# Attention, soft mixture of experts and a gated layer on one core: w_in by column blocks, its product inside the layer

## The chip, the cores and the metric

One core of one Trainium2 chip runs the whole program. The metric is the device time of one execution in microseconds (us), the median of several runs. TensorE (PE), VectorE (DVE), ScalarE (ACT), GpSimd (POOL) and SyncE (SP, which only issues transfers here) work side by side and meet at semaphores.

## The reference

Three parts follow one another; the change touches the second's end and the third.

1. Attention over 2 x 8 heads of 768 rows and 64 columns, with a mask from hash bits. Its result, laid out as x (1536 x 512), feeds the next.
2. A soft mixture of 8 experts with 4 slots each, 32 slots in all: `logits = x @ phi`, weights d (softmax over rows) and c (softmax over slots), `slot_input = d.T @ x`, per expert `relu(slot_input[e] @ w1[e]) @ w2[e]` (512 to 1024 to 512), and `x = c @ slot_out`.
3. A gated layer: `h = x @ w_in` (512 to 2048), `g = h * sigmoid(1.702 h)`, `out = g @ w_out` (2048 to 512).

Everything is fp32. Since x has rank 32 after part 2, the kernel never forms it: with slot_out (32 x 512) it makes `G = slot_out @ w_in` (32 x 2048) once, and then h as c times G.

## The kernel before

The attention and the routing run to about 299 us of the profile and are not touched. From there:

**Experts (L777 to L808, to about 340 us).** TensorE makes for each expert an up product (L786), two transposes (L796) and a down product (L805), up two experts ahead. All three use plain fp32, and the up and down products have stationary operands of 32 columns, so that four of them lie side by side in the array, each writing 32 of the 128 partitions of PSUM. ScalarE takes the hidden rows out (L960), VectorE rectifies them into hid_t (L1154). After the down products of experts 3, 4 and 5 (TURNS) a turn of c is put in: four transposes (L816) turn c, repeated four times over the partitions, into a bank; ScalarE rounds it into c_t (L970), and VectorE replaces the lower 64 partitions by the bank less its rounded value (L1166). So c_t holds rounded values in its first two quarters of 32 partitions and remainders in the last two.

**Rounded operands.** The products of the output layer take operands in a rounded form of fp32 (F32R), which TensorE takes in one pass. A value is split into a rounded part and a remainder, and sums of products of parts stand in for the exact product. g_stack (128 x 2048) holds G's rounded part in quarters 0 and 2 and its remainder in 1 and 3, against c_t's order, so one product over 128 partitions gives all four combinations.

**G (L834 to L849).** acc, the sum of the down products in four quarters, goes through ScalarE (L972), is summed over the quarters and turned by four small products with stack_i (L834) and copied by VectorE into out_t (L1168: 128 x 4 x 32). Then 16 products in plain fp32 (four chunks of w_in's rows, four blocks of 512 columns) make G, the block j in quarter j of bank 5:

```
            for c in in_order:
...
                for j in range(NQ):
                    last = nc.tensor.matmul(ps[j * QUAD:(j + 1) * QUAD, 5, :], out_t[:, c, :],
                                            win_sb(c)[:, j * BANK:(j + 1) * BANK], start=(c == in_order[0]),
                                            stop=(c == in_order[-1]))
```

VectorE rounds it (L1172) and makes the remainder (L1174). place_g (L412) copies a block's rounded part into two quarters of g_stack (ScalarE) and its remainder into the other two (VectorE), 32 partitions each; block 0 before the layer starts, blocks 1 to 3 in the layer's first three steps.

**The output layer (L852 to L887).** 48 steps s: three groups g of 512 rows, 16 blocks fi of 128 columns of h. up(s) (L859) is one product of g_stack and c_t into bank fi % 4, issued three steps ahead. ScalarE makes the sigmoid (L989), VectorE the gate (L1205), its rounding (L1193) and remainder (L1195). Then 12 products (L878, L879, L880; three for each tile tt of 128 rows) add into banks 4 to 7. In the first 16 steps ScalarE also rounds a block of w_out (round_w, L979) and VectorE makes its remainder (split_w, L1181), one step ahead.

**Transfers.** SP issues all of them, in the written order, on one queue. The weights of the experts go through 11 slots of 2 MB; fills 11 to 19 take slots in the order REUSE and wait until the slot's reader is done (hid_ready or down_done). w_in comes in chunks of 128 rows: the fourth early as win_last (1 MB), the first two as fill 16 (2 MB), the third as fill 17 (1 MB); w_out as fills 18 and 19 (2 MB each). The program's instructions stand in the order that is written out for each engine.

The functions that the diff touches, with the profile's line numbers:

Of the kernel before, what the change touches and what calls it, by code (L numbers as in the profile page):

```python
# [36 lines left out]
def kernel_program(nc, q, k, v, proj, phi, w1, w2, w_in, w_out, out):  # L37
# [28 lines left out]
    with ExitStack() as ctx:  # L66
# [74 lines left out]
        win_last = arena[:, W_AT:W_AT + FF]  # L141
# [18 lines left out]
        at[0] = X_AT + 2 * HR + HD  # L160
        g_part = part(2 * FF // NQ).bitcast(F32R).rearrange("p (y n) -> p y n", y=2)
# [22 lines left out]
        g_high = rounded("g_high", ring_at + 4 * SLOT * 4, [P, DEEP, BANK])  # L184
        g_low = rounded("g_low", ring_at + 4 * SLOT * 4 + 4 * DEEP * BANK, [P, DEEP, BANK])
# [43 lines left out]
        win_last_got = sem("win_last_got")  # L229
# [31 lines left out]
        g_steps = sem("g_steps")  # L261
        g_placed = [sem(f"g_placed{y}") for y in range(2)]
# [81 lines left out]
        def win_sb(c):  # L344
            if c == CH - 1:
                return win_last
            return slot[slot_of(WIN0 + c // 2)].rearrange("p (c n) -> p c n", n=FF)[:, c % 2, :]

        def wout_sb(fi):
            return slot[slot_of(WOUT0 + fi // 8)].rearrange("p (f n) -> p f n", n=HD)[:, fi % 8, :]  # L350
# [39 lines left out]
        def fill(eng, n):  # L390
            s = slot_of(n)
            if n < WIN0:
                e, second = divmod(n, 2)
                eng.dma_start(w2_sb(e) if second else w1_sb(e), w2_d[e] if second else w1_d[e])\
                    .then_inc(w_got[s], DMA)
            elif n < WOUT0:
                c = 2 * (n - WIN0)
                chunks = range(c, min(c + 2, CH - 1))
                eng.dma_start(slot[s].rearrange("p (c n) -> p c n", n=FF)[:, 0:len(chunks), :],
                              win_d[:, c:c + len(chunks), :])\  # L400
                    .then_inc(w_got[s], DMA)
            else:
                f = 8 * (n - WOUT0)
                eng.dma_start(slot[s].rearrange("p (f n) -> p f n", n=HD), wout_d[:, f:f + 8, :])\
                    .then_inc(w_got[s], DMA)

        TURNS = (3, 4, 5)

        def place_g(copy, y, j):

            for x in (y, y + 2):
                last = copy(g_stack[x * QUAD:(x + 1) * QUAD, j * BANK:(j + 1) * BANK],  # L412
                            g_part[j * QUAD:(j + 1) * QUAD, y, :])
            return last
# [823 lines left out]
```

## Time and profile before

| | us |
|---|---|
| median of 3 runs | 498.57 |
| lowest, highest | 497.43, 498.71 |
| profiled execution, its own time | 502.64 |
| span of that execution in the profile | 500.8 |

The profiled execution is one run of its own. The span counts from the first to the last instruction recorded; the execution's own time is 1.8 us longer. TensorE's mean granted clock over the span is 0.978 of full.

### The profile page before, as it was taken

The page shows a single profiled execution, that of the slowest core. Times are in us where ns is not written, and L with a number is a line of the kernel's source. Part 1 is how long each engine was busy: PE and PEld are TensorE (multiplying, and loading weights), DVE is VectorE, ACT ScalarE, POOL GpSimd, SP SyncE. Part 2 cuts the span into 40 slices and gives each one's busy share as a digit, 9 for nine tenths or more (in the row PEclk, how much of TensorE's full clock was granted, in tenths as well). Part 3 has the DMA queues.
Part 4 walks back from the last instruction along what each step waited for, and adds up shares of the span by engine and source line. Part 5 has one row for each costly group of instructions (what it writes and reads, how often), then busy time and mean ns, then how long its engine had stood idle before and what let it go on. Part 6 is the DMA issues. An engine that isn't in the chain of part 4 may idle for free.

```text
span 500.8 us, 8465 instructions
## 1 busy us (share of the span) xinstructions
PE 463.7 (93%) x2817; PEld 328.3 (66%) x2817; DVE 292.5 (58%) x582; ACT 229.8 (46%) x476; POOL 108.3 (22%) x194
## 2 busy tenths in 40 slices
PE   3899999999999999999999979967799999999997
PEld 2776666766766667666676634322588888888885
DVE  4477567756666566756665241012998576648661
ACT  1476666666676666666675321101743132112210
POOL 4233245423552255324522000000000000000000
PEclk9999999999999999999999979988799999999999
DMA  6746668666975668656455759999000020002002
GB/s 151 180 127 176 152 172 241 180 177 143 221 216 162 153 192 228 176 162 158 125 190 164 275 198 362 399 409 374 5 0 2 0 85 0 2 11 75 0 0 85
DMA packets 55832, 76.76 MB, mean 153 GB/s; under 512 B 29312, under 2 KB 33280, under 8 KB 55296
## 3 DMA queue, kind: packets, MB, share of 16 engines
q1 hardware_dynamic: 55808, 76.44, 51.0%
q8 instruction: 15, 0.25, 0.2%
q14 instruction: 9, 0.07, 0.0%
HBM read 51.45 MB, written 3.15 MB: 109 GB/s over the span
## 4 chain that ended last, share of the span: by engine, by line
PE 84%; DVE 7%; DMA 6%; ACT 1%; issue 1%; SPq 1%; DVEq 0%; ACTq 0%
PE ps L632 16%; PE ps L656 14%; PE ps L641 11%; PE ps L878 9%; PE ps L879 9%; PE ps L880 9%; DMA ring_lo<-in_moe_w 4%; DVE max_raw L1013 3%; PE ps L618 2%; PE ps L859 2%; PE ps L610 2%; PE ps L786 2%; DVE arena L1007 2%; PE ps L805 1%; PE ps L718 1%
## 5 line engine op out<-in xcount | busy, mean ns | idle before, releaser
L1013 DVE TENSOR_REDUCE max_raw<-ps 128x1 f32<-128x768 f32 x96 | 91.9, 958 | 74.2 <-PE ps L632 71.4
L900 ACT ACTIVATE arena<-ps,neg_max 128x768 f32<-128x768 f32 x96 | 86.6, 902 | 24.6 <-DVE neg_max L1016 24.1
L632 PE MATMUL ps<-stack_b,stack_a 96*128 96x384 f32 (+1 forms) x384 | 95.3, 372 | 1.7 <-ACT arena L900 1.0
L894 ACT COPY arena<-ps 128x384 f32<-128x384 f32 x144 | 64.3, 480 | 68.8 <-PE ps L641 68.8
L632 PEld LDWEIGHTS ps<-stack_b,stack_a 96*128 96x128 f32 (+1 forms) x384 | 65.1, 196 | 39.3 <-issue 36.6
L641 PE MATMUL ps<-ident,arena 128*128 128x128 f32 x576 | 80.5, 276 | 1.0 <-DVE arena L1007 0.6
L878 PE MATMUL ps<-w_high,g_high 128*128 128x512 f32 x192 | 75.8, 395 | 2.9 <-DVE g_low L1195 2.9
L879 PE MATMUL ps<-w_low,g_high 128*128 128x512 f32 x192 | 75.7, 394 | 0.0
L880 PE MATMUL ps<-w_high,g_low 128*128 128x512 f32 x192 | 75.6, 394 | 0.0
L641 PEld LDWEIGHTS ps<-ident,arena 128*128 128x128 f32 x576 | 69.8, 142 | 5.5 <-DVE arena L1007 1.1
L656 PE MATMUL ps<-arena 128*64 128x384 f32 x384 | 72.1, 498 | 0.0
L989 ACT ACTIVATE arena<-ps 128x512 f32<-128x512 f32 x48 | 28.3, 599 | 81.4 <-PE ps L859 81.4
L555 POOL TENSOR_TENSOR high<-arena,ones 128x768 fp32r<-128x768 f32 x15 | 22.0, 1468 | 134.1 <-DVE arena L1025 131.6
L1205 DVE TENSOR_TENSOR arena<-ps,arena 128x512 f32<-128x512 f32 x48 | 33.0, 688 | 21.8 <-ACT arena L989 21.8
L878 PEld LDWEIGHTS ps<-w_high,g_high 128*128 128x128 f32 x192 | 36.6, 191 | 11.0 <-issue 3.3
L880 PEld LDWEIGHTS ps<-w_high,g_low 128*128 128x128 f32 x192 | 36.6, 191 | 7.7
L879 PEld LDWEIGHTS ps<-w_low,g_high 128*128 128x128 f32 x192 | 36.6, 191 | 7.6
L656 PEld LDWEIGHTS ps<-arena 128*64 128x64 f32 x384 | 23.4, 136 | 25.6 <-issue 25.6
L1195 DVE TENSOR_TENSOR g_low<-arena,g_high 128x512 fp32r<-128x512 f32 x48 | 33.2, 693 | 1.7
L610 PE MATMUL ps<-ident,arena 128*128 128x128 f32 x96 | 18.1, 307 | 12.8 <-DMA arena<-in_k 5.0
L558 POOL TENSOR_TENSOR low<-arena,high 128x768 fp32r<-128x768 f32 x15 | 27.3, 1820 | 1.7 <-DMA stack_a<-low 0.5
L1007 DVE COPY arena<-ps 128x384 f32<-128x384 f32 x48 | 26.7, 556 | 0.8 <-PE ps L641 0.4
(119 smaller groups left out, 420.3 us busy)
## 6 DMA issues: line engine op xcount, KB each, us to landing
ring_lo<-in_moe_w SPq DMA_DIRECT2D x12, 1024.0 KB, 5.6
arena<-in_moe_w SPq DMA_DIRECT2D x5, 2048.0 KB, 8.6
ring_lo<-in_moe_w SPq DMA_DIRECT2D x4, 2048.0 KB, 15.8
stack_a<-high SPq DMA_DIRECT2D x32, 192.0 KB, 3.6
stack_b<-high SPq DMA_DIRECT2D x32, 192.0 KB, 3.9
arena<-in_q SPq DMA_DIRECT2D x16, 192.0 KB, 3.6
arena<-in_k SPq DMA_DIRECT2D x16, 192.0 KB, 4.5
arena<-in_v SPq DMA_DIRECT2D x16, 192.0 KB, 2.4
```

The source lines that it names most:

```text
L632: last = nc.tensor.matmul(s_ps[p % 2][:, c, :], a[r][0:used, rows], b[r][0:used, cols], start=(a is stack_a1), stop=(a is stack_a2))
L641: last = nc.tensor.transpose(ring[b][:, j * P:(j + 1) * P], probs[:, p % 2, kt * P:(kt + 1) * P], ident[:, :])
L656: last = nc.tensor.matmul(o_ps[x * D:(x + 1) * D, :], nat_v[:, r, kt, :], probs_t[:, kt, turned(r, x * HALF)[0], :], start=(kt == 0), stop ...
L878: nc.tensor.matmul(ps[:, 4 + tt, :], g_high[:, s % DEEP, rows], w_h, start=(fi == 0), stop=False)
L879: nc.tensor.matmul(ps[:, 4 + tt, :], g_high[:, s % DEEP, rows], w_l, start=False, stop=False)
L880: last = nc.tensor.matmul(ps[:, 4 + tt, :], g_low[:, s % DEEP, rows], w_h, start=False, stop=(fi == FC - 1))
L894: nc.scalar.copy(probs_t[:, b * HALF:(b + 1) * HALF, g, j * P:(j + 1) * P], ring[b].rearrange("p (a s) -> p a s", a=HALF)).then_inc(t_take ...
L900: nc.scalar.activation(probs[:, p % 2, :].rearrange("p (c s) -> p c s", c=2), s_ps[p % 2], ACT.Exp, bias=neg_max[:, r, p:p + 1], scale=SCA ...
L1007: nc.vector.tensor_copy(probs_t[:, HALF:TILES, g, j * P:(j + 1) * P], ring[1].rearrange("p (a s) -> p a s", a=HALF)).then_inc(t_taken[1], 1)
L1013: nc.vector.tensor_reduce(max_raw[:, r, p:p + 1], s_ps[p % 2], axis=AX.XY, op=ALU.max)\
L1195: nc.vector.tensor_tensor(g_low[:, s % DEEP, :], gated[:, s % 2, :], g_high[:, s % DEEP, :], ALU.subtract)\
L1205: nc.vector.tensor_tensor(gated[:, s % 2, :], ps[:, fi % 4, :], sig[:, s % 4, :], ALU.mult)\
```

## The change

w_in is read in four blocks of 512 columns with all its 512 rows (win_first is block 0), each 1 MB, and w_out in four loads of 1 MB, issued in turn behind the last expert's weights. G is made per block: g_parts(j) makes four products, one per chunk of 128 rows, chunk c into quarter c of bank 3, each a sum of its own; ScalarE copies the bank (take_g); g_sum(j) multiplies it with spread, a 128 x 128 matrix of 16 identities of 32 x 32, which adds the four quarters and puts the sum into all four; ScalarE rounds that into g_stack (round_g), and VectorE overwrites the lower 64 partitions with the remainder (low_g). So g_stack now holds rounded values in quarters 0 and 1 and remainders in 2 and 3, and c_t is made to match: rounded in 0 and 2, remainders in 1 and 3, by two subtractions of 32 partitions. Blocks 1 to 3 are made in the layer's first steps: g_parts(j) at the end of step 4(j - 1), g_sum(j) in the middle of the next. h uses three banks instead of four, and up is issued two steps ahead, behind the first three products of a step. spread takes the place of ones, and g_high and g_low move to the slot of w2 of expert 7.

The diff (declarations of semaphores left out, indented eight columns less):

```diff
@@ -138,7 +138,7 @@
 assert Y_AT + SLOT <= ARENA
-win_last = arena[:, W_AT:W_AT + FF]
+win_first = arena[:, W_AT:W_AT + FF]
 at_slot = [ring_lo[:, s, :] for s in range(LO)] + \
@@ -157,8 +157,8 @@
 d_sb = part(NT * SL).rearrange("p (t s) -> p t s", t=NT)
-at[0] = X_AT + 2 * HR + HD
-g_part = part(2 * FF // NQ).bitcast(F32R).rearrange("p (y n) -> p y n", y=2)
+at[0] = X_AT
+g_part = part(BANK)
 sig = arena[:, W_AT:W_AT + 4 * BANK].rearrange("p (w n) -> p w n", w=4)
@@ -181,8 +181,10 @@
 DEEP = 4
-g_high = rounded("g_high", ring_at + 4 * SLOT * 4, [P, DEEP, BANK])
-g_low = rounded("g_low", ring_at + 4 * SLOT * 4 + 4 * DEEP * BANK, [P, DEEP, BANK])
+UPS = 3
+spread = ones[:, :]
+g_high = rounded("g_high", arena_at, [P, DEEP, BANK])
+g_low = rounded("g_low", arena_at + 4 * DEEP * BANK, [P, DEEP, BANK])
 gated = arena[:, Z_AT:Z_AT + 2 * BANK].rearrange("p (w n) -> p w n", n=BANK)
@@ -341,13 +347,21 @@
-def win_sb(c):
-    if c == CH - 1:
-        return win_last
-    return slot[slot_of(WIN0 + c // 2)].rearrange("p (c n) -> p c n", n=FF)[:, c % 2, :]
+def half(s, x):
+    return slot[s][:, x * (SLOT // 2):(x + 1) * (SLOT // 2)]
+def win_at(j):
+    return win_first if j == 0 else half(slot_of(WIN0 + (j - 1) // 2), (1, 0, 1)[j - 1])
+def win_sb(j):
+    return win_at(j).rearrange("p (c n) -> p c n", n=BANK)
+def wout_at(y):
+    return half(slot_of(WOUT0 + y // 2), y % 2)
 def wout_sb(fi):
-    return slot[slot_of(WOUT0 + fi // 8)].rearrange("p (f n) -> p f n", n=HD)[:, fi % 8, :]
+    return wout_at(fi // 4).rearrange("p (f n) -> p f n", n=HD)[:, fi % 4, :]
@@ -389,29 +403,23 @@
     s = slot_of(n)
-    if n < WIN0:
-        e, second = divmod(n, 2)
-        eng.dma_start(w2_sb(e) if second else w1_sb(e), w2_d[e] if second else w1_d[e])\
-            .then_inc(w_got[s], DMA)
-    elif n < WOUT0:
-        c = 2 * (n - WIN0)
-        chunks = range(c, min(c + 2, CH - 1))
-        eng.dma_start(slot[s].rearrange("p (c n) -> p c n", n=FF)[:, 0:len(chunks), :],
-                      win_d[:, c:c + len(chunks), :])\
-            .then_inc(w_got[s], DMA)
-    else:
-        f = 8 * (n - WOUT0)
-        eng.dma_start(slot[s].rearrange("p (f n) -> p f n", n=HD), wout_d[:, f:f + 8, :])\
-            .then_inc(w_got[s], DMA)
+    e, second = divmod(n, 2)
+    eng.dma_start(w2_sb(e) if second else w1_sb(e), w2_d[e] if second else w1_d[e])\
+        .then_inc(w_got[s], DMA)
+def fill_win(eng, j):
+    eng.dma_start(win_sb(j), win_d[:, :, j * BANK:(j + 1) * BANK]).then_inc(win_got[j], DMA)
+def fill_wout(eng, y):
+    eng.dma_start(wout_at(y).rearrange("p (f n) -> p f n", n=HD), wout_d[:, 4 * y:4 * y + 4, :])\
+        .then_inc(wout_got[y], DMA)
+def freed(eng, s):
+    e, second = divmod(s, 2)
+    eng.wait_ge(down_done if second else hid_ready, e + 1)
 TURNS = (3, 4, 5)
-def place_g(copy, y, j):
-    for x in (y, y + 2):
-        last = copy(g_stack[x * QUAD:(x + 1) * QUAD, j * BANK:(j + 1) * BANK],
-                    g_part[j * QUAD:(j + 1) * QUAD, y, :])
-    return last
@@ -493,16 +501,21 @@
     sp.wait_ge(o_ready, HEADS)
-    for n in range(SLOTS - 3, WOUT0 + 2):
+    for n in range(SLOTS - 3, WIN0):
         if n == SLOTS - 1:
         elif n >= SLOTS:
-            e, second = divmod(slot_of(n), 2)
-            sp.wait_ge(down_done if second else hid_ready, e + 1)
+            freed(sp, slot_of(n))
         fill(sp, n)
             sp.wait_ge(o_back, HEADS)
-            sp.dma_start(win_last, win_d[:, CH - 1, :]).then_inc(win_last_got, DMA)
+            fill_win(sp, 0)
+    for n in range(WIN0, WOUT0 + 2):
+        freed(sp, slot_of(n))
+    fill_wout(sp, 0)
+    for j in range(1, NQ):
+        fill_win(sp, j)
+        fill_wout(sp, j)
     for g in range(G):
@@ -836,37 +849,41 @@
     pe.wait_ge(out_t_taken, 1)
-    in_order = (0, 1, 3, 2)
-    for c in in_order:
-        if c == CH - 1:
-            pe.wait_ge(win_last_got, DMA)
-        else:
-            got(pe, WIN0 + c // 2)
-        for j in range(NQ):
-            last = nc.tensor.matmul(ps[j * QUAD:(j + 1) * QUAD, 5, :], out_t[:, c, :],
-                                    win_sb(c)[:, j * BANK:(j + 1) * BANK], start=(c == in_order[0]),
-                                    stop=(c == in_order[-1]))
-    last.then_inc(g_ready, 1)
...
+    def g_parts(j):
+        pe.wait_ge(win_got[j], DMA)
+        if j:
+            pe.wait_ge(g_placed, j)
+        for c in range(CH):
+            last = nc.tensor.matmul(ps[c * QUAD:(c + 1) * QUAD, 3, :], out_t[:, c, :], win_sb(j)[:, c, :],
+                                    start=True, stop=True)
+        last.then_inc(g_ready, 1)
+    def g_sum(j):
+        if j == 0:
+            pe.wait_ge(spread_ready, 1)
+        pe.wait_ge(g_taken, j + 1)
+        nc.tensor.matmul(ps[:, 3, :], spread, g_part, start=True, stop=True).then_inc(g_summed, 1)
...
         g, fi = divmod(s, FC)
-        if s >= 4:
-            pe.wait_ge(gate_ready, s - 3)
+        if s >= UPS:
+            pe.wait_ge(gate_ready, s - UPS + 1)
         if s % NQ == 0 and s < FC:
-            for y in range(2):
-                pe.wait_ge(g_placed[y], s // NQ + 1)
-        nc.tensor.matmul(ps[:, fi % 4, :], g_stack[:, fi * P:(fi + 1) * P], c_t[:, g * BANK:(g + 1) * BANK],
+            pe.wait_ge(g_placed, s // NQ + 1)
+        nc.tensor.matmul(ps[:, s % UPS, :], g_stack[:, fi * P:(fi + 1) * P], c_t[:, g * BANK:(g + 1) * BANK],
                          start=True, stop=True).then_inc(h_ready, 1)
-    AHEAD = 3
+    g_parts(0)
+    g_sum(0)
+    AHEAD = 2
     for s in range(AHEAD):
...
             s = g * FC + fi
-            if s + AHEAD < G * FC:
-                up(s + AHEAD)
             if g == 0:
@@ -881,10 +898,16 @@
                     last.then_inc(y_ready, 1)
+                if tt == 0 and s + AHEAD < G * FC:
+                    up(s + AHEAD)
+                if tt == 1 and s < FC and s % NQ == 1 and s // NQ + 1 < NQ:
+                    g_sum(s // NQ + 1)
             if fi == FC - 1:
...
                 last.then_inc(g_used, 1)
+            if s < FC and s % NQ == 0 and s // NQ + 1 < NQ:
+                g_parts(s // NQ + 1)
@@ -970,12 +993,24 @@
     nc.scalar.copy(acc_sb, ps[:, 7, :]).then_inc(acc_taken, 1)
-    act.wait_ge(g_steps, 1)
-    place_g(nc.scalar.copy, 0, 0).then_inc(g_placed[0], 1)
+    def take_g(j):
+        act.wait_ge(g_ready, j + 1)
+        nc.scalar.copy(g_part, ps[:, 3, :]).then_inc(g_taken, 1)
+    def round_g(j):
+        act.wait_ge(g_summed, j + 1)
+        nc.scalar.copy(g_stack[:, j * BANK:(j + 1) * BANK], ps[:, 3, :]).then_inc(g_rows, 1)
+    take_g(0)
+    round_g(0)
...
-        got(act, WOUT0 + fi // 8)
+        if fi % 4 == 0:
+            act.wait_ge(wout_got[fi // 4], DMA)
         nc.scalar.copy(w_high[fi // 8][:, fi % 8, :], wout_sb(fi)).then_inc(w_rounded, 1)
@@ -986,10 +1021,12 @@
                 act.wait_ge(gate_ready, s - 3)
-            nc.scalar.activation(sig[:, s % 4, :], ps[:, fi % 4, :], ACT.Sigmoid, scale=1.702)\
+            nc.scalar.activation(sig[:, s % 4, :], ps[:, s % UPS, :], ACT.Sigmoid, scale=1.702)\
                 .then_inc(sig_ready, 1)
-            if s + 1 < NQ:
-                place_g(nc.scalar.copy, 0, s + 1).then_inc(g_placed[0], 1)
+            if s < FC - NQ and s % NQ == 2:
+                take_g(s // NQ + 1)
+            if s < FC - NQ and s % NQ == 3:
+                round_g(s // NQ + 1)
             if s + 1 < FC:
@@ -1148,6 +1185,8 @@
         .then_inc(slot_taken, 1)
+    nc.vector.tensor_copy(spread.rearrange("p (j s) -> p j s", j=NQ),
+                          stack_i[:, :].unsqueeze(1).broadcast_to([P, NQ, SL])).then_inc(spread_ready, 1)
     for e in range(E):
@@ -1162,18 +1201,21 @@
             dve.wait_ge(c_high, n + 1)
-            tail = c_t[2 * QUAD:P, n * BANK:(n + 1) * BANK]
-            nc.vector.tensor_tensor(tail, ps[2 * QUAD:P, 6, :], tail, ALU.subtract).then_inc(ct_taken, 1)
+            for x in (1, 3):
+                tail = c_t[x * QUAD:(x + 1) * QUAD, n * BANK:(n + 1) * BANK]
+                last = nc.vector.tensor_tensor(tail, ps[x * QUAD:(x + 1) * QUAD, 6, :], tail, ALU.subtract)
+            last.then_inc(ct_taken, 1)
     dve.wait_ge(out_t_ready, 1)
...
-    dve.wait_ge(g_ready, 1)
-    nc.vector.tensor_copy(g_part[:, 0, :], ps[:, 5, :]).then_inc(g_steps, 1)
-    dve.wait_ge(g_steps, 1)
-    nc.vector.tensor_tensor(g_part[:, 1, :], ps[:, 5, :], g_part[:, 0, :], ALU.subtract).then_inc(g_steps, 1)
-    dve.wait_ge(g_steps, 2)
-    place_g(nc.vector.tensor_copy, 1, 0).then_inc(g_placed[1], 1)
+    def low_g(j):
+        dve.wait_ge(g_rows, j + 1)
+        tail = g_stack[2 * QUAD:P, j * BANK:(j + 1) * BANK]
+        nc.vector.tensor_tensor(tail, ps[2 * QUAD:P, 3, :], tail, ALU.subtract).then_inc(g_placed, 1)
+    low_g(0)
@@ -1199,13 +1241,13 @@
             s = g * FC + fi
+            if s < FC - NQ and s % NQ == 3:
+                low_g(s // NQ + 1)
             dve.wait_ge(sig_ready, s + 1)
                 dve.wait_ge(g_split, s - 1)
-            nc.vector.tensor_tensor(gated[:, s % 2, :], ps[:, fi % 4, :], sig[:, s % 4, :], ALU.mult)\
+            nc.vector.tensor_tensor(gated[:, s % 2, :], ps[:, s % UPS, :], sig[:, s % 4, :], ALU.mult)\
                 .then_inc(gate_ready, 1)
-            if s + 1 < NQ:
-                place_g(nc.vector.tensor_copy, 1, s + 1).then_inc(g_placed[1], 1)
             split_gated(s)
```

## Rows read from the trace of the kernel before

**Rows 1.** The page: busy time of each engine, and the chain's shares by engine.
```profile
PE 463.7 (93%) x2817; PEld 328.3 (66%) x2817; DVE 292.5 (58%) x582; ACT 229.8 (46%) x476; POOL 108.3 (22%) x194
...
PE 84%; DVE 7%; DMA 6%; ACT 1%; issue 1%; SPq 1%; DVEq 0%; ACTq 0%
```

**Rows 2.** Chain that ended last, in order of time: start us, us, what.
```profile
307.82 20.45 DMA ring_lo<-in_moe_w
...
334.71 0.59 ACT c_t L970
...
336.39 3.67 PE ps L805 x32
...
340.09 0.60 ACT arena L972
...
340.82 1.06 PE ps L834 x8
...
342.26 5.38 PE ps L846 x32
...
350.61 0.61 ACT arena L989
...
354.15 0.77 PE ps L878
```

**Rows 3.** Stretches: from:to, length, PE, PEld, DVE, ACT, POOL busy, PEclk, DMA share, GB/s.
```profile
332.20:342.20 10.00, 7.38 (x63) 3.11 (x62) 1.27 (x4) 1.17 (x2) 0.12 (x1) 1.00 1.01 408
342.50:345.50 3.00, 3.00 (x16) 0.65 (x12) 0.00 (x0) 0.00 (x0) 0.00 (x0) 0.50 1.05 386
346.00:348.00 2.00, 1.59 (x16) 0.26 (x8) 0.34 (x1) 0.00 (x0) 0.00 (x0) 1.00 1.05 388
348.00:352.50 4.50, 1.16 (x4) 0.67 (x4) 3.79 (x8) 3.68 (x6) 0.00 (x0) 1.00 0.55 201
...
354.10:359.20 5.10, 5.05 (x12) 4.06 (x13) 4.95 (x10) 4.75 (x9) 0.00 (x0) 0.50 0.00 0
359.50:497.40 137.90, 137.90 (x609) 113.89 (x607) 92.01 (x155) 34.82 (x61) 0.00 (x0) 1.00 0.05 17
```

**Rows 4.** TensorE's groups by form, 328 to 352: line, names, form, count | busy, mean ns.
```profile
L805 PE MATMUL ps<-ring_lo,x_sb 128*32 128x512 f32 x32 | 3.8, 597 | 1.5 <-DVE x_sb L1154 1.5
```

**Rows 5.** Single lines of the kernel: count, duration ns min/median/max, first and last start.
```profile
L878 PE MATMUL ps<-w_high,g_high x192: 389/389/767, 354.1 to 496.6; 128*128 128x512 f32 x192
...
L624 PE MATMUL ps<-v_part,ones x32: 222/248/275, 31.5 to 271.7; 128*128 128x64 f32 x32
...
L1166 DVE TENSOR_TENSOR c_t<-ps,c_t x3: 694/695/695, 320.8 to 335.3; 64x512 fp32r<-64x512 f32 x3
```

**Rows 6.** Timeline of TensorE, three neighbouring pieces of the experts: start us, us.
```profile
307.57 1.91 PE L786 MATMUL ps<-arena,v_part 128*32 128x256 f32 x32
309.41 0.44 PE L796 MATMUL ps<-ident,arena 128*128 128x128 f32 x2
309.78 1.92 PE L805 MATMUL ps<-ring_lo,x_sb 128*32 128x512 f32 x16
```

**Rows 7.** Timeline of VectorE, one step of the output layer and the next's first.
```profile
365.33 0.68 DVE L1181 TENSOR_TENSOR w_low<-ring_lo,w_high 128x512 fp32r<-128x512 f32 x1
...
366.72 0.43 DVE L1193 CAST g_high<-arena 128x512 fp32r<-128x512 f32 x1
367.18 0.69 DVE L1195 TENSOR_TENSOR g_low<-arena,g_high 128x512 fp32r<-128x512 f32 x1
367.79 0.68 DVE L1181 TENSOR_TENSOR w_low<-ring_lo,w_high 128x512 fp32r<-128x512 f32 x1
```

**Rows 8.** Timeline: SP's issue of w2 of expert 7, TensorE's fourth down product.
```profile
313.38 2.84 SPq L394 DMA_DIRECT2D arena<-in_moe_w  x1
...
317.68 1.92 PE L805 MATMUL ps<-arena,x_sb 128*32 128x512 f32 x16
```

**Rows 9.** DMA issues of 312 to 352: KB each, median us to landing.
```profile
arena<-in_moe_w SPq DMA_DIRECT2D x1, 2048.0 KB, 20.3
```

More of the change, by code:

```diff
@@ L228, in kernel_program @@
         w_got = [sem(f"w_got{s}") for s in range(SLOTS)]
-        win_last_got = sem("win_last_got")
+        win_got = [sem(f"win_got{j}") for j in range(NQ)]
+        wout_got = [sem(f"wout_got{j}") for j in range(NQ)]
         xt_ready = sem("xt_ready")
@@ L260, in kernel_program @@
         g_ready = sem("g_ready")
-        g_steps = sem("g_steps")
-        g_placed = [sem(f"g_placed{y}") for y in range(2)]
+        spread_ready = sem("spread_ready")
+        g_taken = sem("g_taken")
+        g_summed = sem("g_summed")
+        g_rows = sem("g_rows")
+        g_placed = sem("g_placed")
         h_ready = sem("h_ready")
```

## The prediction

> **What bounds the kernel now.** I read the page first. TensorE is busy for 463.7 of 500.8 us and holds 84% of the chain that ended last [rows 1], so what counts is TensorE's time and the places where it stands still. Next the chain in order of time around the edited lines [rows 2]. It shows one wait for a transfer, that of a weight block of the experts, until 328.27 (307.82 and 20.45). From there the chain is arithmetic and no transfer of w_in stands in it: the third turn of c_t (ScalarE at 334.71, VectorE behind it) holds back the experts' last products until 336.39, then come acc (340.09), its four small products (340.82) and out_t, the 16 products of w_in (from 342.26, 5.38 us), VectorE's two steps on them, copies into g_stack, ups and the gate, and at 354.15 the first product of the output layer. Third, the stretches [rows 3]: from 359.5 to 497.4 TensorE is busy all of 137.9 us, 609 matmuls at 0.227 us each. A step of 13 takes 2.95 us and nothing waits for anything. So whatever TensorE is given inside this layer lengthens the kernel in full, and whatever is taken away before 354.15 shortens it in full. The edit does both.
>
> **Start of the layer, before.** From 342.26 to 354.15: 11.9 us [rows 2].
>
> **Start of the layer, after.** Only block 0 stands ahead: 4 plain fp32 products (parts), a copy by ScalarE, one 128x128 fp32 product over 512 columns (spread), a rounding copy by ScalarE, a subtraction by VectorE, then up(0), sigmoid, gate, rounding, subtraction. The price of plain fp32: the trace has 32 records for sum_v, which the program issues 16 times [rows 5], so one product is two records. A 512-column fp32 record lasts 597 ns [rows 4], one of the rounded kind 389 ns [rows 5]: 0.21 more, one more pass over the columns, so its pitch is 0.227 + 0.21 = 0.44 us. That agrees with the 16 column-tiled records at 309.78, 1.92 us with the tail [rows 6]: four side by side, four turns of 0.44. Parts are 8 records, 0.87 us; the spread is two records that cannot lie side by side, also 0.87 us. Each has a tail of 0.16 (0.389 less 0.227). Hand-overs are 0.14 to TensorE (340.09 + 0.60 to 340.82 [rows 2]) and 0.03 elsewhere. At the full clock: parts 1.03 + copy 0.59 + 0.14 + spread 1.03 + rounding 0.59 + subtraction 0.69 + 0.14 + up 0.39 + sigmoid 0.60 + gate 0.69 + rounding 0.43 + subtraction 0.69 + 0.14, and some 0.2 of small hand-overs: 7.3 us (ScalarE's from [rows 2], VectorE's from [rows 7], the subtraction of 64 rows from [rows 5]). At 1.2 GHz parts and spread take 0.87 more each, up 0.2: 9.2 us. The clock rows show 0.50 from 342.5 to 345.5, after 2.6 us without work in the ten before, and 1.00 from 346 [rows 3]; parts fall into the first, the spread near its end. I take the middle, 8.3. Gain: 3.6 us, bounds 2.7 and 4.6.
>
> **The blocks inside the layer.** Blocks 1 to 3 put three times parts and spread into TensorE's unbroken stream: 0.87 + 0.87. Parts are column-tiled (32 columns) between products of 128. The experts have the same change [rows 6]: 32 tiled records of 256 columns take 1.84 until a 128-wide product starts (307.57 to 309.41), where four turns of 0.44 are 1.75, and the two 128-wide ones of 128 columns take 0.37 until a tiled one starts, where 2 x 0.11 would do. So 0.09 + 0.15, some 0.25 for both changes. The Trainium skill (TensorEngine Tiling (Array Packing), Key Properties) says a change of tiling mode drains the engine, which speaks against this edit. By that rule, with the tail of 0.16 at each end as the drain, a block would pay 0.32 and the three blocks 6.2 us instead of 5.9. The trace agrees that the change costs something, and has it slightly cheaper. From the rows: 3 x (0.87 + 0.25 + 0.87) = 6.0 us lost, less some 0.1 where weight loads overlap: 5.9. The bound below is a spread at one pass per record (nothing in [rows 4 to 6] has 128 weight columns and 512 moving ones in plain fp32), 4.6; above, 6.7, with drains of 0.32 and some wait on weights.
>
> **The clock in the first step.** TensorE runs at 0.50 from 354.1 to 359.2 [rows 3], after 4.5 us in which four ups (1.16 us) were its only work. Half of the 5.1 us from 354.1 is lost, 2.55. After the edit two ups lie in the some 2.9 us ahead of the first output product, and parts and spread ahead of them: lean, though less long empty. I take the same loss; bounds 2.5 less (no fall) and 1 more (a longer stay, with parts of block 1 in it).
>
> **c_t's turn.** The subtraction, one op of 64 rows at 0.69 us, becomes two of 32 rows, and rows count for nothing beside 512 columns (64 and 128 rows both take 0.69 [rows 5, 7]). The second adds the pitch of 0.61 (367.18 to 367.79 [rows 7]). The third turn stands in the chain [rows 2], and the expert's rectification behind it: +0.6 us. The first two turns end under the wait for the transfer until 328.27 and cost nothing; without that cover they would cost 1.2 more.
>
> **Edits at nothing.** The copy into ones (128x128) runs while TensorE does the first expert product. place_g leaves: 8 copies of ScalarE and 8 of VectorE, those at the start counted above, the rest beside TensorE. In their place come six ScalarE copies and three VectorE subtractions. VectorE needs 2.46 us a step (365.33 to 367.79 [rows 7]) against TensorE's 2.95, so 0.61 once in four steps fits. ups are issued two steps ahead, not three: up(s+2) is followed by 22 products, 5.0 us, before its result is due, and the chain behind it takes 2.6. SP: seven loads of 1 MB follow w2 of expert 7 instead of loads of 2, 1, 2 and 2 MB, the same 7 MB, all behind a wait for the fourth down product. That ended at 319.6, the last w2 issue at 316.2, and such a load lands 20 us after its issue [rows 8, 9], so there is backlog until some 333 and no hole: w_out block 0 lands near 336, due near 348; the last near 351, due ten steps later. If the queue ran dry, 3 us of it would still be covered.
>
> **Sum.** -3.6 + 5.9 + 0.6 + 0 = +2.9 us. The profiled execution's own time is 502.64, 4.1 above the median of 498.57. I add the difference to the median: 501.5. A measurement of this kernel can tell about 0.3%, 1.5 us, from no change.
>
> **Hand-over inside a block (against it, in the forecast).** Let T be the end of parts. ScalarE: copy, round_w, sigmoid, but the rounding needs the spread. TensorE's spread starts after 7 products (T + 1.6) and has ended at T + 2.6; rounding T + 3.2; VectorE T + 4.0; with the hand-over T + 4.1. TensorE reaches up(4) after 9 more products, T + 4.5. Slack 0.4 us.
>
> **Rivals.**
> (a) The hand-over is late: the slack of 0.4 is used up by queueing on ScalarE (it stands in take_g until T, with round_w(3) and sigmoid(3) behind) and on VectorE (low_g stands ahead of gate and split). From 0.4 on each further us is paid three times; a hand-over 1 us late gives 3 x 0.6 = 1.8, 503.3. For it: three engines in strict order; against it: VectorE's half us a step of reserve [rows 7].
> (b) The spread is cheap: at one pass per record 0.43 less in each of four places, 1.7 us: +1.2, 499.8, no change. For it: no row with its form; against it: all rows of plain fp32.
> (c) The other side: the clock stays up. If parts and spread, spaced out from 342.9, keep TensorE at 2.4 GHz until the first output product, the start takes 7.3 and the first step loses nothing: -4.6 + 5.9 + 0.6 - 2.55 = -0.7, 497.9; with (b)'s bound -2.4, faster. It decides from the point where that product starts at 2.4 GHz. For it: 1.59 us of products in 346 to 348 were enough to stay at 1.00 until 352.5; against it: the ups alone were not [rows 3]. The Trainium skill (TensorE: Matmul & The Clock Gate, Part 1) has the throttled clock as the default that activity releases, which would favour the denser start; by that rule the sum is this rival's -0.7, and the trace's 0.50 after lean stretches agrees.
> (d) The transfers come late after all (SP's wait, or blocks of 2 KB rows slower than the rest): ScalarE stands in round_w, some 2 us, 503.5. Nothing in [rows 8, 9] speaks for it, and the rate is 408 GB/s [rows 3].
>
> **How the numbers follow.** Forecast 0.58 (0.55 slower, 0.03 within 0.3%); (a) 0.14, slower; (b) 0.14, of which 0.11 within; (c) 0.12, 0.07 within and 0.05 faster; (d) 0.02, slower. Faster 0.05, same 0.21, slower 0.74. The forecast's own bounds, not all taken together, give +0.5 to +5; (a) and (c) stretch it a little: 498.4 to 504.2.
>
> **What would show it.** Right: from out_t to the first output product 7.3 to 9.2 us instead of 11.9; spread records at 0.44 pitch, 0.87 a product; TensorE without idle from then on, but its stream some 5.9 longer; the third c_t turn 0.6 longer; no wait on a DMA behind 328. Wrong: idle of TensorE ahead of up(4), up(8), up(12) (then (a)), a spread of 0.43 (b), a first step of 3 us (c), ScalarE waiting for w_out (d). A kernel under 497 would mean that the layer's stream had room which [rows 3] do not show.

## The result and the profile after

The changed kernel took 507.44 us (median of 4 runs, 503.86 to 509.59) against 498.64 us for the kernel before (4 runs, 497.43 to 500.09); the ratio is 1.0168, 95% interval 1.0095 to 1.0241. So it is slower, and by more than was forecast (501.5, range to 504.2). Four runs are few for a kernel that scatters like this one: eight more of the changed kernel beside 31 of the kernel before (the first experiment) give 504.53 against 500.18, ratio 1.0104, interval 1.0069 to 1.0139, that is 3.5 to 7.0 us with 5.2 in the middle (4.35 by the medians alone). The ratios leave out the runs of the kernel before that lay more than 1.5% above its fastest (its slow state): two of these 31 (505.19 and 506.04), two of the 32 and one of the 11 in the table below. The first median, 507.44, is on the high side: two of its four executions took over 509 us, and of the ten later ones two did. The sizes below are held against the 5.2 and, piece by piece, against the pair of traces.

The profiled execution's own time is 509.20 us, its span 507.4; before they were 502.64 and 500.8. So the pair of traces differs by 6.6 us. The page of the changed kernel (the rows that answer to [rows 1], and the clock by slices):

```profile
PE 469.3 (92%) x2825; PEld 329.0 (65%) x2825; DVE 293.9 (58%) x580; ACT 229.9 (45%) x476; POOL 108.3 (21%) x194
...
PEclk9599999999999999999999979976899999999999
```

TensorE is busy 5.6 us longer. The 5 in the second digit is a stay at half the clock early in the attention, which the trace before has not (nor has that of the third execution below). It cost nothing that is seen: the two chains stand at 307.80 and 307.82 us at the same wait. But it lowers the mean granted clock, 0.963 here, so that mean says little about the edited part. The chain in order of time, the same view as [rows 2]: start us, us, what.

```profile
328.52 0.04 issue
...
334.90 0.59 ACT c_t L993
...
336.21 0.70 DVE c_t L1206
...
337.28 5.37 PE ps L818 x32
...
344.84 1.44 PE ps L859 x8
...
346.30 0.59 ACT arena L1000
...
347.03 2.06 PE ps L868 x2
...
349.11 0.59 ACT g_stack L1005
...
349.73 0.71 DVE g_stack L1216
...
353.97 0.77 PE ps L895
...
359.55 0.99 PE ps L859 x8
...
362.37 0.86 PE ps L868 x2
363.23 0.23 PE ps L895
```

Four things are to be seen. First, the transfer of the last up weights ends at 328.52 (before: 328.27). Second, behind ScalarE's third c_t copy at 334.90 there is a second subtraction (336.21), and the experts' last products start 2.38 us after that copy, before 1.68. Third, these 32 records take 5.37 us, before 3.67. Fourth, what is called the start below, from the first product that reads out_t (344.84) to the first output product (353.97), is 9.1 us in place of 11.9. The stretches, with the columns of [rows 3]:

```profile
338.80:342.00 3.20, 3.20 (x19) 0.81 (x12) 0.00 (x0) 0.00 (x0) 0.00 (x0) 0.50 1.05 386
345.90:354.00 8.10, 3.65 (x9) 1.06 (x5) 3.38 (x6) 3.80 (x7) 0.00 (x0) 0.50 0.59 217
354.00:359.00 5.00, 5.00 (x12) 3.95 (x13) 4.47 (x8) 0.60 (x1) 0.00 (x0) 0.50 0.01 3
359.50:504.00 144.50, 144.50 (x640) 115.61 (x639) 94.24 (x156) 40.45 (x70) 0.00 (x0) 1.00 0.05 17
```

The last down products ran at half the clock (0.50 in 338.8 to 342), and so did everything from 345.9 to 359. From 359.5 TensorE is busy without a gap, as before, with 640 records in 144.5 us where [rows 3] have 609 in 137.9. What a block of G adds there is seen in TensorE's timeline for block 2 (start us, us, line):

```profile
373.08 0.39 PE L897 MATMUL ps<-w_high,g_low 128*128 128x512 f32 x1
373.40 1.06 PE L859 MATMUL ps<-ring_lo,v_sum 128*32 128x512 f32 x8
374.40 0.50 PE L895 MATMUL ps<-w_high,g_high 128*128 128x512 f32 x1
374.73 0.39 PE L896 MATMUL ps<-w_low,g_high 128*128 128x512 f32 x1
...
375.89 0.40 PE L897 MATMUL ps<-w_high,g_low 128*128 128x512 f32 x1
376.13 1.02 PE L868 MATMUL ps<-arena,ones 128*128 128x512 f32 x2
376.58 0.79 PE L895 MATMUL ps<-w_high,g_high 128*128 128x512 f32 x1
377.21 0.39 PE L896 MATMUL ps<-w_low,g_high 128*128 128x512 f32 x1
```

The products of the layer start every 0.23 us. The one behind 373.08 was due at 373.31. Instead come the parts; the product at 374.40 is followed by the next only at 374.73, 0.33 later, so the stream is back in step 1.19 us late. The spread at 376.13 costs 0.86 in the same way (376.12 due, 376.98 in effect), and with slightly wider pitches around it the distance of two ups becomes 3.87 instead of 2.95, 0.92.

The 6.6 us of the pair, by pieces of the chain: landing of the transfer 0.25; from there to ScalarE's third c_t copy -0.06; c_t 0.70; last down products 1.70; start -2.76 (9.13 for 11.89); and the stream, which is what the stretch from the first output product to VectorE's last copy (at 504.05) is called below: 150.08, before 143.32, so 6.76. That is 6.59.

### The profile page after: what moved, and what is told of

Same layout as the page of the kernel before. It is cut to its first block, busy times and chain, and to the rows that moved or that the text cites. A ratio compares the mean times of both kernels' runs of the same rounds, so it can differ in the third digit from the quotient of the medians.

```text
span 507.4 us, 8487 instructions
## 1 busy us (share of the span) xinstructions
PE 469.3 (92%) x2825; PEld 329.0 (65%) x2825; DVE 293.9 (58%) x580; ACT 229.9 (45%) x476; POOL 108.3 (21%) x194
## 4 chain that ended last, share of the span: by engine, by line
PE 84%; DVE 6%; DMA 6%; ACT 1%; issue 1%; SPq 1%; DVEq 0%; ACTq 0%
PE ps L645 16%; PE ps L669 14%; PE ps L654 11%; PE ps L895 9%; PE ps L896 9%; PE ps L897 9%; DMA ring_lo<-in_moe_w 4%; DVE max_raw L1050 3%; PE ps L876 2%; PE ps L631 2%; PE ps L623 2%; PE ps L818 2%; PE ps L799 2%; DVE arena L1044 2%; PE ps L731 1%
## 5 line engine op out<-in xcount | busy, mean ns | idle before, releaser
L923 ACT ACTIVATE arena<-ps,neg_max 128x768 f32<-128x768 f32 x96 | 86.6, 902 | 24.6 <-DVE neg_max L1053 24.0
L895 PE MATMUL ps<-w_high,g_high 128*128 128x512 f32 x192 | 77.4, 403 | 2.3 <-DVE g_low L1237 2.3
```

Of the source, the lines that this page charges most:

```text
L895: nc.tensor.matmul(ps[:, 4 + tt, :], g_high[:, s % DEEP, rows], w_h, start=(fi == 0), stop=False)
L923: nc.scalar.activation(probs[:, p % 2, :].rearrange("p (c s) -> p c s", c=2), s_ps[p % 2], ACT.Exp, bias=neg_max[:, r, p:p + 1], scale=SCA ...
```

## The experiments

Each is compared with runs of the kernel before on the same chip. Medians and ratios in one place, the reading behind each.

| run | median us (runs) | before us (runs) | ratio, interval |
|---|---|---|---|
| changed kernel again | 504.53 (8) | 500.18 (31) | 1.0104, 1.0069 to 1.0139 |
| no blocks 1 to 3 | 498.99 (10) | 500.18 (31) | 0.9976, 0.9948 to 1.0005 |
| no spread 1 to 3 | 501.56 (10) | 500.18 (31) | 1.0039, 1.0010 to 1.0069 |
| hybrid | 499.04 (12) | 500.18 (31) | 0.9974, 0.9956 to 0.9992 |
| before, filled | 497.34 (12) | 500.77 (32) | 0.9955, 0.9931 to 0.9980 |
| changed, filled | 503.50 (9) | 500.77 (32) | 1.0080, 1.0048 to 1.0112 |
| second hybrid | 497.14 (12) | 500.77 (32) | 0.9952, 0.9923 to 0.9982 |
| second hybrid, filled | 496.09 (12) | 500.77 (32) | 0.9938, 0.9914 to 0.9962 |
| one c_t subtraction | 504.93 (11) | 500.79 (21) | 1.0072, 1.0049 to 1.0095 |
| before again | 500.40 (8) | 500.79 (21) | 1.0004, 0.9967 to 1.0041 |
| swap of the two layouts | 505.90 (6) | 500.78 (11) | 1.0106, 1.0079 to 1.0134 |
| changed kernel, third | 506.56 (2) | 500.78 (11) | 1.0126, 1.0063 to 1.0188 |

**The changed kernel again.** No edit. 

> The changed kernel once more, for its spread. Theory (TensorE's own time): the three blocks cost it 6.4 us, one up more behind the start 0.4, the second c_t subtraction 0.6, and the start gives 2.8 back; that is 4.6, and the clock adds what it happens to add. It expects some 505 to 507 as the median, and a single execution that is longer by 2 to 5 us with a lower mean granted clock. Rival (clock alone): where both kernels have the same mean clock they take the same time.

Its profiled execution took 502.97, 6.2 us less than the first. The median, 504.53, lies just under the 505 to 507 expected. In its chain:

```profile
334.04 3.67 PE ps L818 x32
...
339.90 1.11 PE ps L859 x8
...
341.76 1.11 PE ps L868 x2
...
347.45 0.76 PE ps L895
```

Here the last down products take 3.67 us, and the start is 7.55 us (339.90 to 347.45) with parts and spread at the full clock. From the first output product to VectorE's last copy it is 150.4 us, as in the first trace. So what the executions differ in lies ahead of the stream; the stream is the same. The 6.2 us of span between the two executions are 1.7 of an earlier landing of the last up weights (326.84 for 328.52), 1.6 of the last expert's up product (1.93 for 3.49), 1.7 of the last down products and 1.6 of the start, with the stream 0.3 longer. The clock rival has something for it at first sight: this execution, at a mean granted clock of 0.982, took 502.97, and the kernel before in its first profile, at 0.978, took 502.64. But one pair settles nothing, and the other runs speak against it: at a mean clock of 0.975 to 0.978 the changed kernel took 504.26 and 504.79 us, and the kernel before 499.39 to 501.70 in 17 runs. The filled kernels below settle it.

**Blocks 1 to 3 left out.**

```diff
 def g_parts(j):
...
+    if j:
+        pe.sem_inc(g_ready, 1)
+        return
     for c in range(CH):
...
 def g_sum(j):
...
+    if j:
+        pe.sem_inc(g_summed, 1)
+        return
     nc.tensor.matmul(ps[:, 3, :], spread, g_part, start=True, stop=True).then_inc(g_summed, 1)
```

> Left out: the products (parts and spread) of blocks 1 to 3 of G, the semaphores are set instead, so three quarters of the layer's output come from what the bank holds. Copies of ScalarE and VectorE stay. Theory (TensorE's own time): 6.4 us less than the changed kernel, because nothing covers these products. Rival (hand-over): if the copies' order on ScalarE and VectorE set the pace, the waits stay and less than 2 us goes. Rival (clock): the time stays within 2 us.

By chance its profiled execution had the clock of the first trace of the changed kernel, which makes the two a clean pair:

```profile
337.67 5.37 PE ps L818 x32
...
345.23 1.50 PE ps L862 x8
...
354.42 0.77 PE ps L901
```

The last down products take 5.37 us in both, the start 9.19 (9.13), and from the first output product to the last copy it is 143.69 us against 150.08: 6.4 us, as the theory had it. The median falls by 5.5, by the ratios (1.0104 and 0.9976) it is 6.4. The hand-over rival (less than 2) and the clock rival are out.

**The spread of blocks 1 to 3 left out.** The second half of the edit above. 

> Left out: the spreading product of blocks 1 to 3 alone; ScalarE rounds what the parts left in the bank. Theory (TensorE's own time): 3 x 0.92, 2.8 us less than the changed kernel, the parts' 3.6 stay. If spread were cheap (one pass a record), 1.4. Hand-over: less than 1, since round_g still stands behind take_g.

From the first output product (348.75) to the last copy (495.65) 146.9 us, 3.2 to 3.5 less than the changed kernel's 150.1 to 150.4; the median falls by 3.0. Its first step left 1.2 GHz some 4.1 us behind the first output product, in the first trace of the changed kernel 5.2 us behind it, which is worth some 0.5 of it. That leaves 2.7 us for three spreads, 0.9 a block, as the timeline has it (0.92), and the cheap spread is out.

**Hybrid.** Block 0 as in the changed kernel; blocks 1 to 3 by the products of the kernel before, in the gaps of the start.

```diff
+def g_direct(c):
...
+    for j in range(1, NQ):
+        last = nc.tensor.matmul(ps[j * QUAD:(j + 1) * QUAD, 3, :], out_t[:, c, :], win_sb(j)[:, c, :],
+                                start=(c == 0), stop=(c == CH - 1))
...
 g_parts(0)
+g_direct(0)
 g_sum(0)
+g_direct(1)
+g_direct(2)
+g_direct(3)
```

ScalarE rounds the bank (step 0) and places blocks 1 to 3 in steps 1, 4 and 7, VectorE makes the remainder in step 1 and places it in steps 2, 5 and 8. c_t is in the layout of before, and low_g(0) takes two subtractions. 

> Block 0 of G as in the changed kernel (parts, spread), blocks 1 to 3 as in the kernel before (12 products in quarters of one bank, then place_g), but put into the gaps of TensorE's start, so nothing of G stands inside the layer; c_t in the layout of before with one subtraction, low_g(0) with two. w_in's blocks are read ahead of w_out. Theory (TensorE's own time): the start takes 7.9 to 9.5 us instead of 11.9, the stream has its old length: 2 to 4 us faster than the kernel before, 494 to 497, and more if the fuller start keeps the clock up. Rival (hand-over): VectorE carries 3.2 us more in steps 1 to 8 against a reserve of 0.5 a step and TensorE waits 1 to 2 us: 496 to 499. Rival (clock): no gain, since the clock falls in the start as before.

It takes 0.26% less time than the kernel before: the side was right, the size of 2 to 4 us was not. The start took 8.81 us (342.86 to 351.67), because up(0) stood behind the last nine of the twelve direct products (2.71 us, from 345.84), and the clock fell once more within the first step.

**Second hybrid.** g_direct(3) moved behind the first two ups. 

> As the hybrid, but of the 12 products of blocks 1 to 3 the last three stand behind the first two ups, in the gap ahead of the first output product. In the hybrid up(0) waited for them. Theory: 0.8 us off the start, 7.9 to 8.0 us with the clock up; 498.2 beside 499.0 for the hybrid. Rival: the hand-overs of VectorE take it back, no difference.

Its chain:

```profile
342.00 1.06 PE ps L870 x8
343.06 0.86 PE ps L880 x6
343.92 1.07 PE ps L890 x2
...
345.63 0.68 DVE g_stack L1242
346.33 0.71 DVE g_stack L1242
...
350.27 0.47 PE ps L923
```

The start is 8.27 us; the direct products behind the spread have left the chain and the two subtractions (345.63, 346.33) set it. From there to the last copy it is 141.4 us, against 143.3 before: the first step ran at the full clock, which gives back some 2.4, and two ups more stand in the stream, 0.45. It is 0.48% faster than the kernel before; against the first hybrid that is 1.1 us by the ratios, whose intervals overlap.

**The kernels filled.** Products that nobody reads, put where TensorE waits.

```diff
+def fill_pe(n, bank):
+    for _ in range(n):
+        nc.tensor.matmul(ps[:, bank, 0:P], ident[:, :], ident[:, :], start=True, stop=True)
```

> The kernel before with idle work for TensorE: 12 products of 128x128 over 128 columns ahead of the last expert's up product (a wait for a transfer), 9 behind the products of w_in, 9 ahead of the first output product, all into banks that nobody reads. Theory (TensorE's own time, with the clock as a second part): the clock stays up, from the landing of the last up weights to the first output product it takes some 22.3 us instead of 25.9 and the first step 3 us instead of 5.3; the time falls by 1 to 3 us on average and scatters less. Rival (the fall of the clock is nothing but chance): same time as before, same scatter.

> The changed kernel with the same idle work in its gaps (12, then 2, 5 and 9). Theory: if the 5 us are TensorE's own time, the distance to the kernel before with fillers stays at 4.5 to 5.5 us. Rival (the clock makes the difference): with the clock up in both the distance goes below 2 us.

> The second hybrid with 12 filler products ahead of the last expert's up product and 5 ahead of the first output product. Theory: both parts add up, the start of 8 us and the clock up in it: 1.5 to 3 us below the second hybrid, 495 to 497. Rival (clock is chance): no difference to the second hybrid.

The kernel before gains 0.45%, some 2.3 us, within the 1 to 3 expected. That it scatters less is not shown: its 12 runs lie between 496.56 and 500.02, the 30 without fillers that the ratio uses between 497.16 and 501.78. In its trace the clock is 1.00 from 328.5 to 360, and the stream from the first output product to the last copy is 141.5 us. A transfer is now what ended last ahead of it:

```profile
326.75 20.21 DMA ring_lo<-in_moe_w_out
...
347.04 0.63 ACT w_high L989
...
351.25 0.47 PE ps L888
```

ScalarE's first rounding of w_out waits 0.3 us for the 2 MB load that lands at 346.96; without fillers ScalarE had other work until 349.65 and did not wait. Behind the first output product TensorE waits twice more, each time for VectorE's remainder of the step, which also has the copies into g_stack to do; the first time:

```profile
354.25 0.23 PE ps L866
354.48 0.04 issue
354.51 0.47 PE ps L888
```

Each of the two costs 0.28 us. The changed kernel, which reads 1 MB of w_out first, has no such wait. But with fillers in both, the changed kernel is still longer by 6.2 us in the medians (0.0125 of the time by the ratios), and by 6.2 us in the stream (147.7 against 141.5, the two waits of 0.28 in it). That is more than the 4.5 to 5.5 expected, and far from the rival's 2, and both streams ran at the full clock from their first product. So the clock is not what makes the difference. The second hybrid with fillers is the fastest of all, 496.09 us, 0.62% under the kernel before; it is 1.05 us under the second hybrid without, less than the 1.5 to 3 expected, and the intervals overlap. In its trace the fillers did what they should for the last expert's up product (1.94 us) and the first step (141.4 us of stream), but parts and the first direct products ran at half the clock, so that the start was 9.9 us and not 8.

**One c_t subtraction, and the kernel before again.**

```diff
-for x in (1, 3):
-    tail = c_t[x * QUAD:(x + 1) * QUAD, n * BANK:(n + 1) * BANK]
-    last = nc.vector.tensor_tensor(tail, ps[x * QUAD:(x + 1) * QUAD, 6, :], tail, ALU.subtract)
-last.then_inc(ct_taken, 1)
+tail = c_t[2 * QUAD:P, n * BANK:(n + 1) * BANK]
+nc.vector.tensor_tensor(tail, ps[2 * QUAD:P, 6, :], tail, ALU.subtract).then_inc(ct_taken, 1)
```

> The changed kernel with the one c_t subtraction of 64 rows of the kernel before and the rest as it is, so that c_t's order does not match g_stack's and the layer's output is another. Theory: 0.6 to 0.7 us less than the changed kernel in the chain between ScalarE's third c_t copy and the experts' last products; the median 504 instead of 504.6, below what the runs can tell, so the chain decides. Rival (c_t hidden): the chain keeps its length there.

> The kernel before under the profile once more, to see what differs between two executions of one kernel. Theory (clock as second part): the stretch from the landing of the last up weights to the first output product, 25.9 us in the first profile with the clock at 1.2 GHz in parts of it, comes out between 22.3 and 26 with the share of 1.2 GHz in it; from there to the last product 143 us, or 141 where the first step is at the full clock. Rival: it is 25.9 again and the difference lies elsewhere.

With one subtraction the distance from ScalarE's third c_t copy to the last down products is 1.68 us again (335.45 to 337.13), 0.70 less: the c_t rival (hidden) is out. The ratio, 1.0072, lies 0.3% under the changed kernel's, and the intervals overlap. The kernel before in its second trace:

```profile
326.43 0.04 issue
...
332.94 3.67 PE ps L805 x32
...
338.80 5.38 PE ps L846 x32
...
350.99 0.76 PE ps L878
```

From the landing to the first output product it is 24.6 us (25.9 in the first trace), mostly because the up product of the last expert took 1.93 us for 3.30. Its start was at 1.2 GHz again, 12.19 us. But the execution was 3.1 us shorter than the first, and 1.84 of that lies ahead of this stretch: the transfer landed at 326.43 for 328.27. So theory and rival each have a part.

**Swap of the two layouts.** c_t as in the edit above, and low_g in two subtractions of 32 rows. 

> The changed kernel with c_t in the order of before (one subtraction of 64 rows a turn) and low_g in two subtractions of 32 rows, so that the layer's output is the reference's again. Theory: the second c_t subtraction cost 0.70 us itself and, with the longer gap it makes, let the experts' last down products fall to 1.2 GHz in three of the five traces that had it and in none of the seven that had not (1.7 us each). So they take 3.67 us here, low_g(0) adds 0.7 to the start, and on average some 1 us goes: 503.5 to 504. Rival (the fall there is chance): as the changed kernel, 504.5 to 505.

```profile
334.38 3.67 PE ps L818 x32
...
340.24 1.13 PE ps L859 x8
...
344.82 0.68 DVE g_stack L1215
...
345.52 0.71 DVE g_stack L1215
...
349.75 0.77 PE ps L895
...
361.06 0.11 issue
361.17 0.47 PE ps L876
```

The last down products took 3.67 us, and the start 9.51, so each did what it was to do. But the median is 505.90, not 503.5 to 504, and the ratio is that of the changed kernel. This expectation missed, and the trace shows where. In the start the spread (2.06) and all behind it ran at half the clock. And the stream is 151.2 us long, 0.8 to 1.4 more than in the three traces of the changed kernel, because low_g has two subtractions in the layer too: at up(4), up(8) and up(12) (the first is shown, 361.06) TensorE now waits for the second one, 0.37 us each time. This is the late hand-over of rival (a), in a kernel that adds 0.70 us to the hand-over. As an estimate, 0.70 less 0.37 leaves 0.33 us of slack in the changed kernel, near the 0.4 of the prediction. So what c_t gives back, 0.7 and sometimes 1.7, is taken by 0.7 in the start and 1.1 in the stream.

**The changed kernel a third time.** 

> The changed kernel a third time under the profile. Theory: products in the stream 150 to 150.4 us from the first output product to the last, whatever the clock in the start; the start 7.5 to 9.2 us; the last down products 3.67 or 5.37 us. Rival (hand-over): the stream's length changes from run to run with the order in which ScalarE and VectorE meet.

The stream is 149.8 us (a little under the 150 to 150.4 expected), the start 9.4 (a little above the 9.2), the last down products 5.37. The stream's length over three executions is 150.1, 150.4 and 149.8, and it goes with the time that the first step stayed at half the clock (5.2, 5.9 and some 4.6 us), and no chain shows a wait of TensorE in it: the hand-over rival is out for the changed kernel.

## Why the prediction was wrong, point by point

The direction was right, and so was the main mechanism: work moved into a stream in which TensorE has no gap is paid in full. The sum was too small: +2.9 where the pair of traces shows +6.6 and the larger sample +5.2 (3.5 to 7.0). The step that failed most is the term for c_t's turn: it priced the second subtraction at 0.6 and the clock behind it at nothing, and in the pair the last down products, which follow it, took 1.70 us more at half the clock. Then come three sizes: the start taken at its middle (0.84 of its gain did not come), the stream (6.76 for 5.9, of which 0.4 are ups that the sum has at nothing and 0.5 the blocks), and c_t's own 0.10. With the landing (0.25, and -0.06 behind it) these make the 3.7 us between +2.9 and +6.6. Against the larger sample the three sizes alone are 1.8 of the 2.3 us missing.

**The blocks inside the layer** (5.9 forecast): 6.4. The pair with equal clock shows it (150.08 and 143.69). Parts and the change of tiling cost 1.19 a block where I had 0.87 + 0.25, the spread 0.92 where I had 0.87. The mis-sized terms are small ones: the change of tiling, 0.32 a block for the 0.25 that I had read off the experts' turns (I had set the reading by the drain, 0.32, aside), the spread's 0.05 a block, and 0.1 taken off for overlapping weight loads. The Trainium skill (TensorEngine Tiling (Array Packing), Key Properties) says that a change of tiling mode drains the engine; the 1.19 agrees with four turns of 0.87 in all and two tails of 0.16.

**The ups** (forecast at nothing): 0.4. With AHEAD at two instead of three only two of the first four ups stand in the gap ahead of the first output product, where [rows 2] and the stretch to 352.5 in [rows 3] have four. Two products of 0.23 moved into the stream. With the blocks left out it still took 143.69 where the kernel before took 143.3. I checked the distance of the ups for waits and did not count where they stand.

**The start** (-3.6, bounds -2.7 and -4.6): -2.8 in the first pair, -2.5 to -4.6 over the executions, since it takes 9.1, 7.55 and 9.4 us in the changed kernel and 11.9 and 12.2 in the kernel before. The terms were right to 0.3. What failed is the middle: two of three executions lay at the half-clock end.

**c_t's turn** (+0.6): 0.70 in the chain in each trace with two subtractions. Under it lay what I had not looked for: TensorE's gap there is 2.2 us instead of 1.5, and in four of the six traces with two subtractions the clock fell in the last down products behind it, 5.37 for 3.67 us; in the eight with one it fell in none. That is 1.7 us of the first pair. The gap alone does not decide it: of the five traces with two subtractions and no fillers the two that kept the clock (experiments 1 and 3 of the table) are those in which the transfer of the last up weights landed early, at 326.8 and 326.0, and the three that lost it had it at 328.5 or later; with one subtraction four traces without fillers had it at 328.2 to 328.9 and kept the clock. What it costs on average stays open. One c_t subtraction alone has a ratio 0.3% lower than the changed kernel, 1.6 us, with overlapping intervals, and the swap brings waits of its own.

**The first step at the half clock** (0): 5.1 us of half clock in the first trace of each, as forecast; where the changed kernel's start ran at the full clock, the fall came just then and lasted 5.9 us (347.45 to some 353.3), so the start's gain was partly given back. Where the clock stayed up the stream was 2.4 us shorter: 147.7 for 150.1 in the changed kernel, and 141.5 for 143.3 in the kernel before with two waits of 0.28 in the 141.5. The prediction had 2.55 for it.

**No transfer in the way** (0): right. ScalarE never waited for w_out, and the landing differed by 0.25 us. The rivals: the late hand-over (a) is out for this kernel, TensorE had no gap behind 359.5, but the swap shows that some 0.3 us more would have brought it; the cheap spread (b) is out; (c), the clock staying up, happened in none of the changed kernel's three traces for the first step, and for the start in one; (d) is out.

Summed with the measured sizes: 6.4 + 0.4 + 0.7 - 2.8 = +4.7 and 1.7 on top in the executions in which the down products' clock falls, against 5.2 measured.

## What to carry to other kernels

A shorter way into a stage pays once. Work put into a stream in which the bounding engine has no gap is paid each time. So count what is moved from a gap into the stream, look-ahead products included. The gaps that the short start leaves are the place for that work: the second hybrid does so and beats both kernels by using the old products in them. And when a wait gets longer on an engine whose clock falls in lean stretches, price what follows it at both clocks.

## What the runs showed of the hardware that I had not expected

- The clock's part is large and differs between executions of one kernel: the same 32 records took 3.67 or 5.37 us, the same start 7.55 or 9.4. The kernel before ranged from 496.99 to 503.24 over the 29 runs that the first ratio uses.
- A late transfer cost twice. In the four traces without fillers in which the last up weights landed at 326.0 to 327.9 us, the up product that waited for them took 1.93 us; in the seven in which they landed at 328.2 to 329.0, part of it ran at half the clock and it took 3.2 to 3.64.
- TensorE products that do nothing, put in gaps, made the kernel before 0.45% faster; with them the granted clock was 1.00 from 328.5 to 360. In the changed kernel they did not prevent the fall in the last down products (5.37 us), which have no filler right ahead of them.
- w_in read in rows of 512 columns goes slower than in rows of 2048: in the stretch from 328.5 to 343 the rate is 387 GB/s in the changed kernel (the row below, columns of [rows 3]) and 405 in the kernel before, in both its traces. In the first of these it is 412 from 335 to 340, with w_in on its way, and 387 from 342 to 346, with w_out, whose rows have 512 columns too. No run changed the row length alone. Nothing waited for it here.

```profile
328.50:343.00 14.50, 11.85 (x88) 4.18 (x88) 1.67 (x4) 1.28 (x3) 0.12 (x1) 0.77 1.05 387
```
